# State increments as products 64 and 48 columns of keys wide, and wider idle products, in a linear-attention and two-network kernel

## The reference, cut to what matters

```python
# q, k, v, f_logit: (batch 4, heads 8, seq 768, head_dim 48)
f = 1.0 / (1.0 + np.exp(-f_logit))
for t in range(S):
    state = f[:, :, t, :, None] * state + np.einsum('bhd,bhe->bhde', k[:, :, t], v[:, :, t])
    y[:, :, t] = np.einsum('bhd,bhde->bhe', q[:, :, t], state)
x = y, as (batch * seq = 3072 tokens, heads * head_dim = 384)
h = x @ moe_w_in            # 384 -> 2048
x = np.maximum(h, 0) ** 2 @ moe_w_out          # 2048 -> 384
h = x @ moe2_w_in
x = (h * np.tanh(np.log1p(np.exp(h)))) @ moe2_w_out
```

## Time and profile before

| | |
|---|---|
| median of 3 runs | 886.29 us |
| lowest, highest | 885.81, 890.02 us |
| the profiled execution's own time | 886.69 us |
| its span (first to last instruction) | 885.0 us |
| TensorE busy | 874.3 us, 99% |
| VectorE, ScalarE busy | 597.2 us, 594.8 us (67% each) |
| granted TensorE clock, mean | 1.0 |

### The profile page before, as it was taken

The page is one execution under the profiler, slowest core; times in us unless marked ns, Lnnn a source line. Parts: engine busy times, 40 slices in busy tenths (PEclk is TensorE's granted clock), DMA queues, the critical chain, the costliest instruction groups (busy, mean ns, idle before and its releaser), DMA issues.

```text
span 885.0 us, 16260 instructions
## 1 busy us (share of the span) xinstructions
PE 874.3 (99%) x6282; PEld 725.3 (82%) x6282; DVE 597.2 (67%) x1054; ACT 594.8 (67%) x1026; POOL 62.0 (7%) x71
## 2 busy tenths in 40 slices
PE   8899999999999999999999999999999999999998
PEld 7788888888888888888788888888888888888886
DVE  6879545445544444342244799999898898898886
ACT  6776655564546555544566787888887887877874
POOL 0222111111111111110000000000000000000000
PEclk9999999999999999999999999999999999999999
DMA  9644221122212111100233201001001001000100
GB/s 255 203 148 128 76 81 44 44 81 65 66 45 80 44 44 57 46 13 1 92 96 100 90 19 37 37 0 37 37 1 37 36 1 37 36 0 1 36 1 36
DMA packets 25090, 50.64 MB, mean 57 GB/s; under 512 B 2674, under 2 KB 3442, under 8 KB 25010
## 3 DMA queue, kind: packets, MB, share of 16 engines
q1 hardware_dynamic: 25010, 49.56, 18.0%
HBM read 40.11 MB, written 9.44 MB: 56 GB/s over the span
## 4 chain that ended last, share of the span: by engine, by line
PE 98%; DMA 1%; issue 0%; SPq 0%; ACT 0%; DVE 0%; ACTq 0%
PE ps L1069 45%; PE ps L1086 44%; PE ps L1043 2%; PE ps L1013 2%; PE ps L1039 2%; PE ps L991 1%; PE ps L1059 1%; DMA work<-fkq 1%; SPq L284 0%; PE ps L988 0%; PE ps L997 0%; SPq L297 0%; ACT work L497 0%; ACT work L538 0%; SPq L306 0%
## 5 line engine op out<-in xcount | busy, mean ns | idle before, releaser
L1069 PE MATMUL ps<-xs,w_hi 128*128 128x512 f32 x1152 | 359.3, 393 | 1.0 <-issue 1.0
L1069 PEld LDWEIGHTS ps<-xs,w_hi 128*128 128x128 f32 x1152 | 213.0, 188 | 45.0 <-issue 1.6
L1086 PE MATMUL ps<-g_hi,w_lo 128*128 128x512 f32 x576 | 224.1, 389 | 0.0
L1069 PE MATMUL ps<-xs,w_lo 128*128 128x512 f32 x576 | 224.1, 389 | 0.0
L1086 PE MATMUL ps<-g_hi,w_hi 128*128 128x512 f32 x576 | 224.1, 389 | 0.0
L1086 PE MATMUL ps<-g_lo,w_hi 128*128 128x512 f32 x576 | 224.1, 389 | 0.0
L829 DVE TENSOR_TENSOR g_lo<-gb,g_hi 128x512 fp32r<-128x512 f32 x96 | 68.1, 709 | 215.6 <-ACT gb L564 215.6
L559 ACT ACTIVATE rb<-ps 128x512 f32<-128x512 f32 x96 | 57.3, 597 | 161.0 <-PE ps L1069 161.0
L1069 PEld LDWEIGHTS ps<-xs,w_lo 128*128 128x128 f32 x576 | 108.1, 188 | 22.6
L1086 PEld LDWEIGHTS ps<-g_hi,w_hi 128*128 128x128 f32 x576 | 108.1, 188 | 22.5
L1086 PEld LDWEIGHTS ps<-g_hi,w_lo 128*128 128x128 f32 x576 | 108.1, 188 | 22.4
(11 more groups left out here) (82 smaller groups left out, 750.6 us busy)
## 6 DMA issues: line engine op xcount, KB each, us to landing
work<-fkq SPq DMA_DIRECT2D x68, 224.0 KB, 3.7
stage<-w SPq DMA_DIRECT2D x24, 384.0 KB, 3.1
work<-v_tok SPq DMA_DIRECT2D x22, 256.0 KB, 3.9
x_scratch<-yo SPq DMA_DIRECT2D x6, 768.0 KB, 3.8
xs<-x_scratch SPq DMA_DIRECT2D x6, 768.0 KB, 4.4
out<-work SPq DMA_DIRECT2D x17, 256.0 KB, 2.1
yo<-w SPq DMA_DIRECT2D x8, 384.0 KB, 4.6
work<-f_tok SPq DMA_DIRECT2D x4, 224.0 KB, 3.5
```

Of the source, the lines that this page charges most:

```text
L1069: ins = nc.tensor.matmul(bank, w[:, f, k * P:(k + 1) * P], xs[:, half, part, k, :], start=k == 0 and i == 0, stop=k == KT - 1 and i == 2)
L1086: ins = nc.tensor.matmul(ps[:, 5 + d, :], w[:, f, cols], g[:, slot, :], start=f == 0 and i == 0, stop=f == NF - 1 and i == 2)
```

## The change

In increments, four products per pair (32, 32, 32 and 16 columns of keys) become two (64 and 48 columns, ROWS), with the same 48 moving columns. Every output element is the same sum as before. The idle products take the identity repeated by a broadcast as their moving operand, up to 384 columns in one product: six products of 128 columns become two of 384, and three become one.

```diff
@@ -34,7 +34,7 @@
     WF = 2 * DM
     NT = NF * NCH
     AHEAD = 4
-    IDLE = [6, 3]
+    IDLE = [(3, 3), (3,)]
     LIMIT = 8.0e16
     BOUND = 1.0e18
     CAP = 1.0e17
@@ -1053,10 +1053,9 @@
                 else:
                     pe.wait_ge(s_["r1_ready"], begin[j + 1] + 1)
                 for n in range(NP):
-                    for i in range(4):
-                        lo, hi = Q * i, min(Q * i + Q, R)
-                        v0, v1 = VALUES[i // 2]
-                        ins = nc.tensor.matmul(ps_kv(j)[lo:hi, n, :], key_rows(j)[:, n, lo:hi], v_rows(j)[:, 2 * n + i // 2, v0:v1],
+                    for par, (lo, hi) in enumerate(ROWS):
+                        v0, v1 = VALUES[par]
+                        ins = nc.tensor.matmul(ps_kv(j)[lo:hi, n, :], key_rows(j)[:, n, lo:hi], v_rows(j)[:, 2 * n + par, v0:v1],
                                                start=True, stop=True, skip_group_check=True, tile_position=(0, lo))
                 ins.then_inc(s_["kv_done"], 1)
 
@@ -1144,9 +1143,10 @@
...
-            def idle_products(count, bank):
-                for i in range(count):
-                    nc.tensor.matmul(ps[:, bank, 0:P], ident[:, :], ident[:, :], start=True, stop=True, skip_group_check=True)
+            def idle_products(widths, bank):
+                for n in widths:
+                    nc.tensor.matmul(ps[:, bank, 0:n * P].rearrange("p (n t) -> p n t", t=P), ident[:, :],
+                                     ident[:, :].unsqueeze(1).to_broadcast([P, n, P]), start=True, stop=True, skip_group_check=True)
 
             pe.wait_ge(s_["const_ready"], 4)
             idle_products(IDLE[0], 6)
```

## The result

The changed kernel takes 890.54 us (median of 6 runs, 889.54 to 891.82) against 886.66 us of the kernel before (median of 6, 885.81 to 890.02): a ratio of 1.0039 with a 95% interval of 1.0022 to 1.0056, so 3.5 us more (2.0 to 5.0); the two medians lie 3.9 us apart. By the bound of 0.5% that is "same", which had 0.92; but it is a true loss, and 890.54 lies over the top of the range, 890.0. The profiled execution took 891.82 us with a span of 890.1 us, 5.1 us more than the span before.

The account below looks back on a forecast made before the run. TensorE, busy for 99% of the span, was taken to bound the kernel. +2.1 us for the jobs, -0.5 for the opening and 0 for the idle products gave +1.6, so 887.9 us from the median 886.29; range 885.2 to 890.0.

Parts of the forecast that it names:

- the sum: Whole kernel: +2.1 us for the jobs, -0.5 for the opening, 0 for the idle products, together +1.6 us.
- Increments, the work itself: Increments of each job: streamed columns set the pace, so the block keeps its 0.36 us, less 0.02 us saved.
- the 0.5 us of gain in the opening: Opening on TensorE: shifted waits for instructions let values(3) and what follows move up, -0.5 us, bounds 0 and -1.9.
- my upper bound of 0.42 us: Increments of a job: 16 records at the 26 ns a record of scores (L1013) take 0.42 us, 0.06 more.
- The new change of width: Values into increments: 64 wide blocks behind 32 wide ones cost 0.15 us a job, bounds 0.10 and 0.15.
- rival 1: Increments: records set the pace, 16 in place of 32, giving -3.1 us, 883.2 us; chance 0.04.
- rival 2: Increments: blocks of 64 columns do not run side by side, giving +7.7 us, 894.0 us; chance 0.04.
- The issue gaps: Two TensorE waits in the opening, 0.37 and 1.55 us, for the next instruction packet, one per 126 or so products.
- The idle products: Start of the opening: the new form takes the same stretch and raises the clock at the same time, 0 us.
- The branch: The 1.0 us wait for instructions before L1069, behind flag_ready: left as it is, bounds -1.0 and +1.0 us.

Follow-up runs that it names:

- e5: Kernel before with the 64 and 48 wide increments, each product cut into two of 24 moving columns with the same weights loaded again; ratio 1.0128.
- e7: Kernel before with the 64 and 48 wide increments alone, with 64 moving columns in place of 48; ratio 1.0040.
- e3: Kernel before with increments in two blocks of 48 columns of keys per pair of heads, old idle products; ratio 1.0027.
- e6: Kernel before with its narrow increments (32, 32, 32 and 16 columns), each product cut into two of 24 moving columns; ratio 1.0110.
- e9: Kernel before with increments of pairs 1 and 3 in 64 and 48 wide blocks, pairs 0 and 2 narrow, in turn; 896.17 us, ratio 1.0113.
- e10: Kernel before with increments of pairs 2 and 3 in 64 and 48 wide blocks, pairs 0 and 1 narrow; 889.55 us, ratio 1.0041.
- e4: Kernel before with increments of pair 3 alone in 64 and 48 wide blocks, pairs 0 to 2 narrow; ratio 1.0037.
- e2: Kernel before with the wide idle products alone, increments as before; 885.86 us, ratio 0.9994.
- e1: Kernel before with the 64 and 48 wide increments alone, idle products as before; 891.00 us, ratio 1.0048.
- e8: Kernel before without any idle products; 886.70 us, ratio 0.9993.

## Why the prediction was wrong

The step that failed is the first of the sum, **"Increments, the work itself"**: "A job after the change is again 4 x 2 groups of 48 columns [...] 8 x 45 = 0.36 us". A group of a 64 and a 48 wide block streams its 48 columns in 45 ns but takes 56 to 61 ns, and this time goes with the columns of weights and not with the moving ones: e5 shows 56 ns with half the moving columns, e7 the same time with a third more, e3 0.09 us less a job with 48 wide blocks. So the block takes 0.59 - 0.10 = 0.49 us. That is 0.13 us more for each of 16 jobs, 2.1 us where the sum had -0.3: 2.4 us beside the 2.6 between 887.9 and 890.5. The other parts nearly cancel, which is luck: the change of width cost 0.5 us less than forecast, the 0.5 us of gain in the opening did not show, and the kernel before has a median of 886.66 in six runs, 0.4 over the 886.29 that the sum started from.

The row I leaned on could not show it. L988 also loads 64 columns, but its 112 moving columns take 95 ns, so a load of 56 to 61 ns is hidden behind them. A row was there: half the products of scores (L1013) stream 64 columns through 64 wide blocks, in groups of four blocks. I divided its 0.83 us by 32 records, 26 ns, and took 16 of those. But a pair is a group, not two quarters of one. Read by groups, 0.83 us less 0.15 for the change of width less 4 groups of 128 columns at 109 ns leaves 0.24 us for the other 4: 61 ns a group, 0.49 us for 8, as measured. This is hindsight, and it hangs on the price of the change: with 0.12 it is 69 ns. But either figure says that my upper bound of 0.42 us was too low, and the range with it.

The Trainium skill has this rule: TensorE: Matmul & The Clock Gate, "LDWEIGHTS (loading the stationary operand)", says that a weight load takes its columns divided by 1.2 in nanoseconds; estimates by it are 53 ns at 64 columns, 40 at 48, 27 at 32. The traces come near for the pace of a group at 64 (56 to 61 ns) and lie above it at 48 (49 ns in e3, where streaming takes 45) and at 32 (36 ns in e6). By it the pair would have been bound by its weights, and I had not weighed it.

Point by point:

- **The new change of width** was right in mechanism and a little dear: 0.12 us in the changed kernel (0.99 against 0.87), 0.13 in e9 against e10, forecast 0.15. e4 shows it with a quarter of the slower block, e9 and e10 by itself. The 0.15 came from a block of L1043 with another width both ahead and behind, and was put down to one change. The sum had 16 x 0.15 = 2.4 us of it, measured 1.9. In the opening I left out a second change: increments(0) is followed by values again, so it takes 0.59 us (23.42 to 24.01) where it took 0.36, 0.23 more and not the 0.13 that I gave it.
- **Records do not set the pace** of the new blocks (rival 1): half as many took longer. **Blocks of 64 columns do run side by side** (rival 2): streamed one after the other, the blocks of a job would take 0.72 us, 0.36 more. The slowdown is 0.13, a third of that, and its cause is another, but on the side that rival 2 named; its threshold, 0.15 us a job, was nearly reached.
- **The issue gaps** sit at a fixed count of instructions, as worked out from the earlier trace rows: the second moved by 12 records in e2 and by 16 in e1, exactly what each removes. Counted from TensorE's first record, the first gap stands behind 219 in the profiles before, e3 and e10, and the second behind 345 in those before, e1, e2, e3 and e9. In the changed kernel 345 falls where I said, with 5 records of values(3) left, but no gap is there. What the shift gains was not settled. The network started at 27.20 and 27.83 us in those two profiles and at 29.26 in the changed kernel's, where loads came later and the clock fell. e2 has the shift of 12 records and is not measurably faster; its interval allows a gain of 1.3 us at most, so my -0.5 is neither shown nor excluded.
- **The idle products** cost nothing that can be told in their new form (e2), and e8 shows that here they are worth nothing. That the first ones ran at 1.2 GHz I took from their pace of 0.22 us a record; the granted clock in the profiles reads 1.00 there, so the level itself is not shown. That the clock fell at 13.6 us in the profile of the changed kernel doesn't need their new form: the profile of e5, with the old ones, reads 0.50 from 13.0 to 15.0 us, behind a wait of 1.37 us for the same logarithm.
- **The branch**: 1.0 us became 1.3 in the changed kernel and 1.6 in e1, inside its bounds of +-1.0.

The sum with measured terms is 16 x (0.12 + 0.13) = +4.0 us with nothing for the opening, against 3.9 between the medians.

## What to carry to other kernels

Products on strips of the array have two candidates for their pace, the columns they stream and the columns of weights they load. Here, in fp32, four strips of 32 with 48 moving columns took 45 ns a group and two of 64 and 48 took 56 to 61: fewer, wider blocks with few moving columns turned a time that was hidden into the bound. Read such a pace by group of strips that run side by side, never by record, and take it from a row where the suspected bound is not covered by the other. And count the changes of block width in a burst: each cost 0.12 to 0.13 us here, more than the 0.02 us of work a job that was to be saved.

## What the runs showed of the hardware that was not expected

- The pace of a group of column strips in fp32 against the columns of weights: 56 to 61 ns at 64 (with 24, 48 and 64 moving columns), 49 ns at 48 (48 moving columns), 36 ns at 32 (24 moving columns, and there a least time for each record would fit as well).
- The granted clock can fall within the opening for some 4 us (0.55 from 13.6 to 17.4), after waits of 0.78 and 1.36 us among short blocks, in some executions of one kernel and not in others, and the median doesn't show it. Waits alone don't decide: e3 waited 0.84 and 1.49 us at the same two places, and its clock stayed at 1.00. In the profiles of e5, e6 and e9 it fell to 0.50 for some 3 us as the network began, which put job 4 of each 1.6 us further behind the start of the network than in the others.
- A kernel without any idle products at the start was as fast as one with nine of them (0.9993).
